# Loading the local v of a pair of heads in four DMAs instead of nine

## The reference, cut to what matters

```python
    q_d = q.reshape(B, H, Sd, factor, D).mean(axis=3)      # factor 4; the same for k and v
    out_d = sm_attn(q_d, k_d, v_d)                         # pooled attention
    out_up = np.repeat(out_d, factor, axis=2)
    mask = np.abs(pos[:, None] - pos[None, :]) < factor    # local attention: a band of 7 positions
    scores = np.where(mask, scale * np.matmul(q, k.transpose(0, 1, 3, 2)), -1000000000.0)
    ...
    out_local = np.matmul(attn, v)
    return (out_up + out_local).astype(np.float32)
```

## Time and profile before

| | |
|---|---|
| median of 3 runs | 877.24 us (877.23 to 878.68) |
| the profiled execution | 878.17 us, its span 876.3 us |
| PE busy | 822.3 us (94%) |
| POOL, DVE, ACT busy | 459.7 us, 403.8 us, 307.4 us |
| DMA queue of SP (q1) | 82896 packets, 34.67 MB |
| attention stage | from 0 to about 159 us of the span |

### The profile page before, as it was taken

One profiled execution on the slowest core, in us unless ns is written; L12 is line 12 of the kernel. 1 busy time (PEld: TensorE's weight loads), 2 busy tenths in 40 slices (PEclk: granted clock), 3 DMA queues, 4 the chain that ended last, 5 costly groups with the idle time before them and its releaser, 6 DMA issues.

```text
span 876.3 us, 17594 instructions
## 1 busy us (share of the span) xinstructions
PE 822.3 (94%) x5522; PEld 713.7 (81%) x5523; DVE 403.8 (46%) x746; ACT 307.4 (35%) x661; POOL 459.7 (52%) x492
## 2 busy tenths in 40 slices
PE   5999998279979999999999999999999999999996
PEld 5888786168858888888879989999898998989995
DVE  3877776564535546554653333242242333233231
ACT  2666565413133432343224223233223323223231
POOL 5886878478878866786645323223214223222322
PEclk9999999789999999999999999999999999999999
DMA  7467686547766644764443002001000100100000
GB/s 167 112 157 178 153 192 176 139 137 222 226 175 202 179 148 143 222 194 148 139 137 114 8 1 73 1 1 47 28 1 36 36 0 24 48 0 3 34 1 37
DMA packets 109416, 88.51 MB, mean 101 GB/s; under 512 B 67329, under 2 KB 81153, under 8 KB 109377
## 3 DMA queue, kind: packets, MB, share of 16 engines
q10 hardware_dynamic: 23040, 41.95, 16.1%
q1 hardware_dynamic: 82896, 34.67, 15.2%
q0 software_dynamic: 3440, 11.38, 3.9%
HBM read 72.87 MB, written 15.10 MB: 100 GB/s over the span
## 4 chain that ended last, share of the span: by engine, by line
PE 72%; SPq 7%; POOL 7%; issue 6%; DMA 4%; DVE 2%; ACT 1%; ACTq 0%; POOLq 0%; DVEq 0%
PE tp L1275 11%; PE tp L1277 11%; PE tp L1276 11%; PE pt L1277 5%; PE pt L1276 5%; PE pt L1275 5%; SPq L371 4%; PE xo L1275 4%; PE xo L1277 4%; PE xo L1276 4%; POOL wts L505 3%; PE sc L1276 3%; PE sc L1277 3%; SPq L367 3%; PE sc L1275 3%
## 5 line engine op out<-in xcount | busy, mean ns | idle before, releaser
L634 POOL TENSOR_TENSOR act_s<-act_f,act_s 128x384 fp32r<-128x384 f32 x96 | 97.4, 1017 | 278.6 <-ACT act_s L818 278.5
L505 POOL TENSOR_TENSOR wts<-stage,wts 128x512 fp32r<-128x512 f32 x160 | 204.7, 1301 | 70.2 <-ACT wts L726 63.6
L726 ACT CAST wts<-stage 128x512 fp32r<-128x512 f32 x160 | 98.5, 621 | 205.4 <-DMA stage<-in_moe_w 89.9
L1275 PE MATMUL tp<-x2T,wts 128*128 128x384 f32 x384 | 130.7, 340 | 0.0
L816 ACT ACTIVATE clamped<-clamped,mhalf 128x384 f32<-128x384 f32 x96 | 59.2, 617 | 199.0 <-DVE clamped L1088 199.0
L1277 PE MATMUL tp<-x2T,wts 128*128 128x384 f32 x384 | 128.9, 336 | 0.0
L1276 PE MATMUL tp<-x2T,wts 128*128 128x384 f32 x384 | 128.7, 335 | 0.0
L1088 DVE TENSOR_SCALAR clamped<-tp 128x384 f32<-128x384 f32 x96 | 53.5, 557 | 149.4 <-PE tp L1277 149.4
L1092 DVE SCALAR_TENSOR_TENSOR act_f<-tp,clamped 128x384 f32<-128x384 f32 x96 | 53.5, 557 | 66.3 <-ACT clamped L816 66.3
L1277 PE MATMUL pt<-wts,act_s 128*128 128x512 f32 x192 | 75.3, 392 | 0.0
L1276 PE MATMUL pt<-wts,act_s 128*128 128x512 f32 x192 | 75.2, 391 | 0.0
(11 more groups left out here) (194 smaller groups left out, 1451.0 us busy)
## 6 DMA issues: line engine op xcount, KB each, us to landing
stage<-in_moe_w ACTq DMA_DIRECT2D x128, 256.0 KB
y_rows<-xg SPq DMA_DIRECT2D x21, 260.0 KB
vw<-in_v SPq DMA_DIRECT2D x144, 36.0 KB
x<-y_rows SPq DMA_DIRECT2D x6, 780.0 KB, 4.4
qn<-in_q SPq DMA_DIRECT2D x32, 144.0 KB, 3.5
kn<-in_k SPq DMA_DIRECT2D x32, 144.0 KB, 3.5
v<-in_v SPq DMA_DIRECT2D x16, 288.0 KB
x_nat<-xb SPq DMA_DIRECT2D x16, 288.0 KB, 3.3
```

Of the source, the lines that this page charges most:

```text
L505: pool.tensor_tensor(wts[:, par, 1, cols], stage[:, n % STG, :], wts[:, par, 0, cols], ALU.subtract).then_inc(lo_done, 1)
L634: pool.tensor_tensor(act_s[f % 4][:, 1, :], act_f[f % 4][:], act_s[f % 4][:, 0, :], ALU.subtract).then_inc(act_lo, 1)
L726: act.copy(wts[:, par, 0, n * CH:(n + 1) * CH], stage[:, n % STG, :]).then_inc(hi_done, 1)
L1275: pe.matmul(o, stationary(0), moving(0), start=start, stop=False)
```

## The change

`load_v` issues four DMAs for a pair instead of nine: for each head one with the seven inner windows (72 x 7 rows of 256 bytes) and one with the two outer ones (72 x 2 rows of 256 bytes). The source patterns are written by hand, as overlapping windows can't be had by slicing. The rows read, the bytes and the places where they land are the same, and PE waits for 4 x 16 instead of 9 x 16 for each pair.

```diff
-    v_h = v.rearrange("b h s d -> s (b h) d")
+    v_mid = bass.AP(tensor=v.tensor, offset=WSTART[1] * D, ap=[[D, W], [BQ * D, NB - 2], [S * D, B * H], [1, D]])
+    v_end = bass.AP(tensor=v.tensor, offset=0, ap=[[D, W], [WSTART[NB - 1] * D, 2], [S * D, B * H], [1, D]])
...
         def load_v(m, j):
-            for t in range(NB):
-                sp.dma_start(vw[j % 2][:, t, :].rearrange("p (h d) -> p h d", h=2),
-                             v_h[WSTART[t]:WSTART[t] + W, bass.ds(2 * m, 2), :]).then_inc(v_loaded[j % 2], 16)
+            for h in range(2):
+                for part, src in ((slice(1, NB - 1), v_mid), (slice(0, NB, NB - 1), v_end)):
+                    sp.dma_start(vw[j % 2][:, part, D * h:D * h + D], src[:, :, 2 * m + h, :]).then_inc(v_loaded[j % 2], 16)
...
         def local_values(m, par, k2):
-            pe.wait_ge(v_loaded[par], 16 * NB * (k2 + 1))
+            pe.wait_ge(v_loaded[par], 64 * (k2 + 1))
```

## The result

| | before | changed |
|---|---|---|
| median | 877.24 us (875.92 to 878.68, 4 runs) | 871.18 us (869.81 to 871.91, 4 runs) |
| ratio, 95% interval | | 0.9916 (0.9888 to 0.9944) |
| the profiled execution | 878.17 us, span 876.3 us | 871.54 us, span 869.7 us |

The changed kernel is faster. The forecast was 872.1 us, a ratio of 0.9941. The median of the runs lies 0.9 us under it, at the low end of the forecast's own range (871.2 to 873.6) and inside the wider one (870.9 to 874.8). But 877.24 times the measured ratio is 869.9 us, which is 1.0 us under the low end of the wider range. The interval of the ratio still holds 0.9941, so by these times alone the miss isn't clear of the scatter. The direction and the mechanism held; the profiled execution gained 6.63 us where 5.10 were forecast.

A forecast was written before the change was run, and what follows sets the result against it. The prediction took SP's DMA issues to bound the attention pairs; 2.51 + 2.59 = 5.10 us off the profiled 878.17 gave 873.1, so 872.1 us for the median, own range 871.2 to 873.6, widened to 870.9 to 874.8.

The forecast's parts named there:

- The bound: Attention pairs, 40 to 118 us: SP's DMA issues, 9.0 to 9.2 us a pair against PE's 8.29, make the others late.
- Steps 1 and 2: SP's v loads: nine issues of 4.44 us a pair go, four of 2.5 us (2.0 to 3.6) come.
- Step 3, the steady pairs: PE between 89.13 and 133.09 us: five pairs at 8.29 take 41.45 us instead of 43.96, gain 2.51 us.
- Step 3, the end of the stage: End of attention: PE's waits of 1.04 us at 143.15 and 1.55 us at 147.54 both go, gain 2.59 us.
- When v4 is issued and used: v4 loads in the steady pairs: POOL wants v4 8.5 us after its issue; slowest landing 6.4 us, so no wait.
- Step 4, DMA: DMA engines: same bytes, 6.4 us a pair on each of 16, 7.2 us on the busy ones, hidden under PE's 8.29.
- the first pairs start on q and k, issued ahead of all v, so nothing changes there: Start of attention: the first pairs were claimed to gain nothing, 0 us.
- A (no change): SP's issues: packets, not instructions, limit SP, so four loads last as long as nine; 877.2 us, 8 in 100.
- B (half): End of attention: v4 still lands late, only the steady pairs gain, 2.51 us; 874.7 us, 8 in 100.
- C (slower): SP's v loads: the two 504-row loads hold SP longer than the nine did; 881 us, 3 in 100.
- D (the first weight load lands sooner): Weight load at 159.04 us, 3.50 us long, lands in 2.4 us: 1.1 us more gain; 871.0 us, 5 in 100.

The follow-up runs named there:

- e4: Changed kernel with the inner windows cut into three or four DMAs a head, nine v loads a pair: 876.89 us, ratio 0.9993 to the kernel before.
- e5: Changed kernel with the inner windows of each head in two DMAs, six v loads a pair: 871.12 us, ratio 0.9931 to the kernel before.
- e8: Changed kernel with the inner windows of each head in five DMAs, twelve v loads a pair: 892.76 us, ratio 1.0179 to the kernel before.
- e11: Kernel before, no edit, profiled a second time: 873.42 us in one run, beside 873.63 for the kernel before on that chip.
- e3: Changed kernel with nine v loads each for the first two pairs, the new ones for the others: 871.76 us, ratio 0.9931 to the kernel before.
- e1: Changed kernel once more, no edit, 5 rounds: 871.39 us, ratio 0.9936 to the kernel before.

## Why the prediction was right, and where it was not

- **The bound.** Right, and shown: SP's issues, and their number (e4, e5, e8). Between 40 and 142 us SP went from no wait to 12 waits for PE's L1195. The prediction's reading of 9.0 to 9.2 us for SP's pair holds for single pairs only; from 67.36 to 129.56 us its v loads begin 8.4 to 9.6 us apart, 8.89 us on average. The gain was worked out from PE's starts, so this changed nothing in the sum.
- **Steps 1 and 2, the cost of the issues.** 4.44 us fell to 1.85, where 2.5 was taken and 2.0 was the low end. A v load with 504 rows costs SP no more than one with 144; the four took 0.46 us each. The term was too large by 0.65 us a pair, and that did no harm, as SP had time to spare either way. Part of the saving came back, which wasn't foreseen: from 40 to 120 us the median issue of `kn` grew from 0.494 to 0.756 us, and the four q and k issues of a pair from 2.51 to 2.96 us on average. Why is not shown.
- **Step 3, the steady pairs.** 2.51 us forecast, 2.54 measured; the other two traces of the kernel before make it 2.8 and 1.8 (102.32 and 101.26 less 99.50).
- **Step 3, the end of the stage.** 2.59 us forecast, 2.31 measured, and 1.2 and 1.8 against the other two traces (23.15 and 23.74 less 21.96). The two waits went as described. I wrote that I counted no more than PE's own waits, but not that one could come in their place: with POOL no longer late, PE reaches the transposes of rows before DVE has emptied the bank, 0.77 us at 139.94. The kernel before has the same wait, 0.60 us, in e11, where PE doesn't wait for POOL there.
- **When v4 is issued and used.** 8.5 us from issue to use was forecast; it is 8.3 to 9.6 us (issued at 81.98, used at 90.26; issued at 122.77, used at 132.37).
- **Step 4, DMA.** Right as to the mean: a share of 0.77 (89.2 to 115.9 us) at 8.3 us a pair is 6.4 us on each engine, the value that was worked out, and no transfer became late. The 7.2 us on the twelve busier engines were not measured.
- **The step that failed** is "the first pairs start on q and k, issued ahead of all v, so nothing changes there". As to the change it held (e3, e11). As to the forecast it didn't; the term was put at 0 and measured 1.50 us: the sum was made against one execution of the kernel before, whose first 31 us held a late full pace of TensorE and a stretch at half clock, which another execution doesn't have. The two profiled executions differ by 1.50 us there, about the whole excess over 5.10, and the timed runs of one kernel scatter over several us (27 runs of the kernel before, 873.18 to 882.66). I gave the range bounds for the costs of the change and none for that. Both its ends should have been some 1.5 us further out, as the slow start can fall to either kernel (e1). That the slow start fell to the kernel before in the first pair of traces was chance, as far as the five traces of the two kernels show. Whether the four timed runs of each kernel lay low for the same reason no run shows.
- **The rivals.** A (no change), B (half) and C (slower) are excluded, by the interval of the ratio and by the waits. D (the first weight load lands sooner) gave 871.0 us, which is nearest to the median, but not by its mechanism: that load took 3.27 us in the chain after, 3.50 before, 0.2 us where D wanted 1.1.

## What to carry to other kernels

Count the DMAs that a queue issues in one round of a loop: where their issue time exceeds the round of the engine that should be the bound, fewer DMAs with more rows each pay, down to the point where the queue has time to spare, and no further (six loads were as good as four). A queue without a single wait in its list is the sign of it: between 40 and 142 us SP had none with nine or twelve loads, 9 with six and 12 with four. Before a forecast of less than one per cent, look in the trace for stretches in which the clock was at half, and widen the range on both sides by what they are worth.

## What the runs showed that was not expected

An issue of v costs SP about the same, 0.46 to 0.50 us with its address work, for 72 to 504 rows of 256 bytes. But rows aren't all: the q and k loads with 576 rows took 0.63 us each on average from 40 to 120 us, and 0.74 us in the changed kernel. TensorE's granted clock fell to 0.50 in the first 26 us in 9 of the 14 traces, and in some and not in others of one and the same kernel (kernel before: 19 to 22 us in two traces, never in e11; changed kernel: never in the first, 18 to 23 us in e1), and the start of pair 1 moved between 29.5 and 31.05 us in these. Its cause wasn't found.
